# An attention and two-mixer kernel: finishing additions spread over the second mixer, angle products between its halves, the first result ahead of the token sums, two half blocks, and a later hold on GpSimd

## What is computed

```python
attn_out = local_and_global_attention(q, k, v)        # 8 heads of 64, window 96, 8 global keys
x = attn_out.transpose(0, 2, 1, 3).reshape(B, S, 512)
# first mixer
h  = np.maximum(x.transpose(0, 2, 1) @ w_tok1, 0.0) @ w_tok2     # 768 -> 256 -> 768
u  = x + h.transpose(0, 2, 1)
x2 = u + np.maximum(u @ w_ch1, 0.0) @ w_ch2                      # 512 -> 1536 -> 512
# second mixer
theta = x2 @ w_theta
y   = einsum('ts,bsd->btd', w_tok_r, x2 * cos(theta)) + einsum('ts,bsd->btd', w_tok_i, x2 * sin(theta))
u2  = x2 + y
out = u2 + np.maximum(u2 @ w_ch, 0.0)
```

## Time and profile before

| | us |
|---|---|
| median of 3 runs (lowest, highest) | 514.46 (514.01, 514.79) |
| profiled execution, its own time | 514.55 |
| span of the profiled execution, first to last instruction | 512.8 |
| PE busy in it | 491.1 (96%) |
| DVE busy | 326.4 (64%) |
| POOL busy | 265.7 (52%) |
| ACT busy | 192.9 (38%) |
| mean granted PE clock | 0.993 of 2.4 GHz |

### The profile page before, as it was taken

How to read it: one execution, slowest core, us unless ns; L and a number is a source line. 1 busy time by engine, 2 the same in 40 slices (tenths; PEclk the granted TensorE clock), 3 DMA queues, 4 the chain that set the end, 5 groups by cost and what they waited for, 6 DMA issues and landing times.

```text
span 512.8 us, 8394 instructions
## 1 busy us (share of the span) xinstructions
PE 491.1 (96%) x2917; PEld 445.3 (87%) x2917; DVE 326.4 (64%) x797; ACT 192.9 (38%) x413; POOL 265.7 (52%) x315
## 2 busy tenths in 40 slices
PE   7999999999999999998899999994999999999997
PEld 5999999898999999797799989883778899888897
DVE  6998998577434353587423346898587684664452
ACT  6999899454111131154111114342232140321130
POOL 3575566599589884069998882473450130000040
PEclk9999999999999999999999999997999999999999
DMA  6897775422222331103143241223001221000002
GB/s 231 316 310 239 230 221 132 133 82 84 65 83 81 98 115 54 42 0 122 43 111 118 78 128 61 93 93 102 23 21 36 69 82 63 0 1 0 2 31 93
DMA packets 27083, 49.81 MB, mean 97 GB/s; under 512 B 3360, under 2 KB 17696, under 8 KB 27040
## 3 DMA queue, kind: packets, MB, share of 16 engines
q1 hardware_dynamic: 27040, 49.26, 30.6%
HBM read 39.81 MB, written 3.15 MB: 84 GB/s over the span
## 4 chain that ended last, share of the span: by engine, by line
PE 84%; POOL 5%; DVE 5%; issue 3%; DMA 1%; ACT 1%; POOLq 0%; DVEq 0%
PE bank L323 61%; PE bank L1758 7%; PE bank L1486 5%; PE bank L1516 4%; PE bank L1519 3%; POOL wsplit L710 3%; PE bank L1500 2%; PE bank L1498 2%; POOL wsplit L704 1%; DMA wraw<-weights 1%; DVE split L1279 1%; DMA counts<-both_counts 1%; DVE bank L1308 1%; PE bank L1526 0%; DVE act_raw L1209 0%
## 5 line engine op out<-in xcount | busy, mean ns | idle before, releaser
L323 PE MATMUL bank<-wsplit 128*128 128x512 f32 (+2 forms) x816 | 149.0, 338 | 1.7 <-DVE bank L1297 1.7
L323 PEld LDWEIGHTS bank<-wsplit 128*128 128x128 f32 x816 | 134.4, 188 | 15.7 <-POOL wsplit L710 1.1
L710 POOL TENSOR_TENSOR wsplit<-wraw,wsplit 128x512 fp32r<-128x512 f32 (+1 forms) x77 | 100.4, 1305 | 39.4 <-ACT wsplit L883 33.8
L323 PE MATMUL bank<-wsplit,zs 128*128 128x512 f32 (+1 forms) x576 | 103.2, 338 | 0.0
L323 PEld LDWEIGHTS bank<-wsplit,zs 128*128 128x128 f32 x576 | 89.6, 188 | 14.1 <-issue 0.2
L778 POOL TENSOR_TENSOR split<-act_raw,split 128x384 fp32r<-128x384 f32 x12 | 12.5, 1075 | 106.4 <-ACT split L995 106.4
L323 PE MATMUL bank<-split,wsplit 128*128 128x384 f32 x276 | 55.1, 342 | 3.3 <-POOL wsplit L710 1.6
L652 POOL TENSOR_TENSOR wsplit<-qk_raw,wsplit 64x256 fp32r<-64x256 f32 x46 | 38.0, 827 | 33.9 <-DVE wsplit L1038 33.5
L323 PEld LDWEIGHTS bank<-split,wsplit 128*128 128x128 f32 x276 | 46.8, 188 | 5.9 <-issue 2.5
L704 POOL CAST wsplit<-wraw 128x512 fp32r<-128x512 f32 (+1 forms) x59 | 36.1, 613 | 28.6 <-PE bank L323 19.2
L323 PE MATMUL bank<-wsplit,tile 128*128 128x512 f32 x144 | 37.6, 412 | 9.6 <-issue 9.3
(11 more groups left out here) (126 smaller groups left out, 749.3 us busy)
## 6 DMA issues: line engine op xcount, KB each, us to landing
wraw<-weights SPq DMA_DIRECT2D x28, 512.0 KB, 3.4
qk_raw<-qk SPq DMA_DIRECT2D x23, 528.0 KB, 4.5
wraw<-weights SPq DMA_DIRECT2D x8, 768.0 KB, 4.0
vt<-v SPq DMA_DIRECT2D x10, 520.0 KB, 4.7
xT<-turned SPq DMA_DIRECT2D x64, 48.0 KB, 2.0
out<-act_raw SPq DMA_DIRECT2D x16, 192.0 KB, 1.9
xT<-turned_early SPq DMA_DIRECT2D x16, 96.0 KB, 2.5
xT<-wraw SPq DMA_DIRECT2D x32, 48.0 KB, 2.0
```

The lines of the kernel that those rows point to most:

```text
L323: mm = pe.matmul(dst, lhs(a), rhs(c), start=first and i == 0, stop=last and i == 2, skip_group_check=True)
L710: ins = pool.tensor_tensor(dst[:, cols], src[:, cols], hi[:, cols].bitcast(F32), ALU.subtract)
```

## The change

Five edits of order. The number and sizes of the instructions stay the same, on every engine; nothing is computed otherwise.

1. *Finishing additions.* Of batch 1's eight, three stay where they were; the other five go behind the low part of the first half of tile 2 (`z_to_lo(2, 0)`).
2. *Angle products.* In batch 0, `angles(g+2)` goes from ahead of `mix(g)` to between its halves.
3. *First result.* On DVE, `result_to_lo(0)` goes ahead of the first token sums, and the next result follows two sums later; on ACT, result i+1 is rounded ahead of sums 2i and 2i+1. Result 3 goes behind the last two `find_sum`.
4. *Two half blocks.* Sum t = 4 goes to banks 0 and 1. Of pair 0's blocks, d = 2 and 3 come first, and of each only the part of 512 columns (banks 2 and 3, which then wait for no sum) stands behind product 0 of pair 1; their parts of 256 columns stand behind product 1.
5. *GpSimd's hold.* POOL's wait for `x2_done` goes from ahead of chunk 16 to behind its combinations and roundings, ahead of its subtractions.

```diff
-            return bank[{1: 4, 3: 0, 2: 4, 4: 2}[t] + kk][:, 0:SC]
+            return bank[{1: 4, 3: 0, 2: 4, 4: 0}[t] + kk][:, 0:SC]
...
                 round_in_pieces(mixes(n, 0, 3, MIXES), sums)
+                if n == PAIR_F + 1:
+                    pool.wait_ge(x2_done, NC * KD)
                 link(rest_in_pieces(mixes(n, 1, 0, 3), raw[:, 0:3 * 2 * P], mixes(n, 0, 0, 3)))
...
-                        if n == PAIR_F + 1:
-                            pool.wait_ge(x2_done, NC * KD)
                         split_first(n, raw).then_inc(w_ready, 1)
...
-                for i, (f, c) in enumerate(REGULAR):
+                def result_to_hi(i):
+                    f, c = REGULAR[i]
                     act.wait_ge(r1_ready, b * PRODUCTS + i + 1)
                     act.activation(r1_at(b * PAIR_F, f, 0, c * SC, SC), bank[6 + i % 2][:, 0:SC],
                                    ACT.Relu).then_inc(r1_hi, 1)
+
+                result_to_hi(0)
+                for i in range(len(REGULAR)):
+                    if i + 1 < len(REGULAR):
+                        result_to_hi(i + 1)
                     sum_to_hi(2 * i)
                     sum_to_hi(2 * i + 1)
...
                         dve.wait_ge(t_hi, b * SUMS + 5 + kk)
+                        dve.wait_ge(t_lo, b * SUMS + 3 + kk)
+                        dve.wait_ge(t_raw, b * SUMS + 5 + kk)
                         src, raw_u, op = t_psum(2, kk), u_raw[:, 2 + kk], ALU.subtract
...
+                result_to_lo(0)
+                for i in range(len(REGULAR)):
+                    find_sum(2 * i)
+                    find_sum(2 * i + 1)
                     if i < 2:
-                        sum_to_lo(2 * i)
-                        sum_to_lo(2 * i + 1)
-                    elif i == 2:
-                        sum_to_lo(4)
-                    else:
-                        sum_to_lo(5)
-                        find_sum(6)
-                        find_sum(7)
-                        sum_to_lo(6)
-                        sum_to_lo(7)
+                        result_to_lo(i + 1)
+                    elif i == 3:
+                        result_to_lo(3)
+                    sum_to_lo(2 * i)
+                    sum_to_lo(2 * i + 1)
...
             z_to_lo(1, 0)
             tile_to_lo(B * T + 3)
-            for i in range(2 * KD):
+            for i in range(3):
                 finish_x2(B - 1, i)
...
                     if g >= 2 and not (b and s == 0):
                         z_to_lo(g, 0)
+                    if g == 2:
+                        for i in range(3, 2 * KD):
+                            finish_x2(B - 1, i)
...
-                def block(i, f, d):
+                def first_block(i, f, d, at):
                     n = b * PAIR_F + i
                     first, last = i == 0 and f == 0, i == PAIR_F - 1 and f == 0
-                    if d == 0:
+                    if d == at:
                         wait_weight(pair_in_order(b, i, 1))
                         pe.wait_ge(r1_lo, b * PARTS + 2 * NC * i + (3 + f if i == 0 else 4 - f))
-                    if first:
-                        pe.wait_ge(t_lo, b * SUMS + 5 + d)
-                        pe.wait_ge(t_raw, b * SUMS + 7 + d // 2)
-                    three(pe, bank[d][:, :], lambda a: second_at(n, a, f * DM + d * P, P),
-                          lambda a: r1_at(n, f, a, 0, 512), first, last)
+                    if first and d < 2:
+                        pe.wait_ge(t_lo, b * SUMS + 7 + d)
+                    return three(pe, bank[d][:, :], lambda a: second_at(n, a, f * DM + d * P, P),
+                                 lambda a: r1_at(n, f, a, 0, 512), first, last)
+
+                def rest_of_block(i, f, d):
+                    n = b * PAIR_F + i
+                    first, last = i == 0 and f == 0, i == PAIR_F - 1 and f == 0
+                    if first and d == 2:
+                        pe.wait_ge(t_lo, b * SUMS + 6)
+                        pe.wait_ge(t_raw, b * SUMS + 8)
                     mm = three(pe, bank[4 + d // 2][:, d % 2 * 256:(d % 2 + 1) * 256],
...
+                    if i == 1:
+                        blocks = blocks[2:4] + blocks[0:2] + blocks[4:]
...
-                block(i - 1, *blocks[2 if ahead else 0])
+                    if i == 1:
+                        first_block(0, *blocks[0], 2)
+                        first_block(0, *blocks[1], 2)
+                    else:
+                        block(i - 1, *blocks[2 if ahead else 0])
                     pe.wait_ge(p1_copied, m + 1)
                     product(i, 1, 6, quarter(2, 0), True)
-                    block(i - 1, *blocks[3 if ahead else 1])
+                    if i == 1:
+                        rest_of_block(0, *blocks[0])
+                        rest_of_block(0, *blocks[1])
+                    else:
+                        block(i - 1, *blocks[3 if ahead else 1])
...
                     mm.then_inc(z_used, 1)
+                    if b == 0 and i == 0 and s + 2 < T:
+                        angles(g + 2)
...
                     g = b * T + s
-                    if b == 0 and s + 2 < T:
-                        angles(g + 2)
```

9 lines of the change are left out of this document (5 added, 4 removed).

## The result

The kernel after took 503.19 us (median of 4 executions, 501.59 to 503.63) against 514.62 us for the kernel before, measured on the same chip: a ratio of 0.9771, with a 95% interval of 0.9746 to 0.9797. That is 11.4 us less; forecast were 9.2 us and 505.3 us.

The account below looks back on a forecast made before the run. The prediction took PE to bound the kernel, busy 491.1 of 512.8 us. Gains of 6.4 + 1.2 + 1.6 = 9.2 us took the profiled 514.55 to 505.35, 505.3 against the median; range 502.8 to 508.5.

Parts of the forecast that it names:

- What bounds the kernel: Whole span: PE busy 491.1 of 512.8 us, so only its gaps and slow stretches can give time.
- Edits 1 and 2, the work: Second mixer's start on PE: 12 halves and four angle products take 62.1 us, against 71.0 before.
- Edits 1 and 2, the waits: Second mixer, PE waiting for DVE at tiles 3 and 4: 2.1 to 4.4 us, taken as 2.5.
- two before POOL comes back, 0.9 us, three beside it, 1.75 + 2 x 1.44, to 361.4: DVE's five moved additions, from 355.8: two at full pace, three slowed by POOL, ending at 361.4.
- rival A: Second mixer: DVE keeps up, fewer instructions meeting POOL, waits near nothing; 502.8, up to 504 us; chance 0.15.
- Rival C: Clock falls in or after the new 2.7 us wait ahead of mix(0), costing 1.8 us: 507.1; chance 0.07.
- Edits 3 and 4: First mixer, first result and half blocks: 0.7 us gained in batch 1 and 0.5 in batch 0, 1.2 together.
- Edit 5: First mixer, batch 1: chunk 20 ready earlier, PE's whole wait of 1.61 us goes; gain 1.6 us.
- Rival D: At chunk 20 another wait (a load) replaces the hold and PE still stands: 506.9 us; chance 0.04.
- Rival E: Slower or level: clock falls ahead of mix(0) and stays low through short waits; 515.5 us; chance 0.05.

Follow-up runs that it names:

- both mixer edits: Kernel before with only five finishing additions moved back and angle products placed between the halves of the mixes; 506.83 us, ratio 0.9828.
- the hold alone: Kernel before with only POOL's wait for x2_done moved behind chunk 16's combinations and roundings; 512.51 us, ratio 0.9953.
- the first-mixer edits: Kernel before with only the first result ahead of the sums and two half blocks ahead of the copy; 513.92 us, ratio 0.9976.
- the last kernel: Kernel after with ACT's copy earlier, tile 2's angle product first, tile 5's behind tile 3's product, additions behind tile 3's low halves; 498.54 us, ratio 0.9675.

## Why the prediction was right, and where it was not

The time fell inside the range and 2.1 us under the forecast. By its steps:

- **What bounds the kernel** held: all but 0.8 us of the span's 13.0 came out of PE's gaps and slow matmuls in the four places named.
- **Edits 1 and 2, the work** held to 0.1 us: 62.1 forecast, 62.2 measured, 2.56 us of new wait ahead of it against 2.7. DVE was laid out almost to the row: the moved additions were put at 355.8 and POOL's return at 356.7, and with both edits alone they came at 355.85 and 356.94.
- **Edits 1 and 2, the waits** is the term that was mis-sized, 2.5 us for none. The step that failed is "two before POOL comes back, 0.9 us, three beside it, 1.75 + 2 x 1.44, to 361.4". All five took 2.29 and ended at 358.1. That 5.6 us were forecast and the run that puts all five behind POOL's start took 5.71 is chance: the forecast had two of the five clear of POOL, and by its prices, 1.75 and 1.44, five beside POOL would take 7.8. Its price held for the two beside subtractions (1.78 and 1.77), while beside casts the three took 0.8 each. And the price depends on who was there first: the prediction took POOL's arrival as the moment from which DVE pays, and it was POOL that paid. So rival A came about in the profiled execution, by another way than it named: not fewer meetings, but meetings that DVE won; the sign named for A, additions of under 1 us beside a working POOL, is in the trace (0.46). With the additions behind POOL's start, the executions at full clock were 2.1 to 2.2 us longer, near the 2.5 forecast: this supports that the waits would have come, had POOL been first.
- **The clock** was the other error, of the opposite sign. Rival C, at 0.07, happened, by the mean clocks, in three of four executions of after and in three of five with both mixer edits; of the six traces with a wait of 2.56 to 2.60 ahead of `mix(0)`, five show the fall. Its price was about right: 1.8 forecast, 503.2 - 501.6 = 1.6 and 506.9 - 505.0 = 1.9 measured between executions, 1.3 to 1.5 on the traces. The argument against it (the clock had held for 5.0 us of idling before) drew a rule from one execution: in the same gap of 7.8 us it fell 2.3 us after PE had stopped in the trace of the hold alone, and 2.4 us after in that of the first-mixer edits. The two errors leave 8.9 - 1.6 = 7.3 us in the median against 6.4 forecast; that they nearly cancel is luck.
- **Edits 3 and 4**: 1.55 us measured in the profiles, 1.2 forecast. The wait for result 0 (0.37, forecast 0.3) and the work ahead of the copy held. With edits 3 and 4 alone PE resumed product 1 at 239.08 against 240.48, 1.4 us earlier, of which 0.2 was there before any edit, 0.65 stems from batch 0 and 0.54 from batch 1; forecast were 0.5 and 0.4. Alone, the gain was nearly lost to the clock, a way in which neither forecast nor rivals had it.
- **Edit 5**: 1.6 forecast, 1.8 on both traces, 2.3 by the time of the edit alone (interval 1.7 to 3.2). POOL's wait, 11.02 us, is what it was to be (near 11). The wait row of 1.61 counts only the idle matmul engine; from row to row the place cost 3.87 us before and 2.10 without the wait, 1.77. Rival D didn't come about.
- **The edits together**: the three groups alone gave 2.3 + 7.9 + 0.9 = 11.1 us, together 11.4. Within the intervals the groups add up, though edit 5 also protects what edits 3 and 4 gain. Within the mixer group they overlap nearly whole, which the prediction, having priced both edits as one, didn't say.
- Rival E found no support: in every trace the clock was full again within 5 us of PE's going back to work.
- **What no term covers**: 0.6 of the 13.0 us of span lie at the start and the end, outside all edits, so that much of the 2.1 us below the forecast is put down to the executions and not to the change.

What stays open: what decides, from one execution to the next, whether the clock falls in a wait of 2 to 3 us. The runs show only where it did.

## What to carry to other kernels

Lay out by hand both the engine that waits and the one that releases, and ask of every wait that you cover how much slack the next release has: here covering 2.56 us of wait gained next to nothing (0.4 us by the medians, inside the noise), since the releasing engine had 0.9 us left. Two edits that lengthen the same distance are worth one of them; time the pair with one taken back before keeping both. And when a copy stands in a queue behind work that waits for another engine, as ACT's did behind the last sums, moving it ahead is a few lines and was worth 3.7 us here, more than edits 3, 4 and 5 by their own runs (0.9 and 2.3).

## What the runs showed of the hardware that was not expected

**The shared port goes by who holds it.** Three additions that met a working POOL took 4.92 us in the kernel after too (from 335.82), whereas the five back to back took 2.30 with POOL's piece starting among them. They were followed without a break by a low half:

```profile
354.05 0.68 DVE L1249 TENSOR_TENSOR zs<-zb,zs 128x512 fp32r<-128x512 f32 x1
```

POOL's piece, 352.89 to 355.88, would have needed 1.35 us, so it began in fact at about 354.5 (worked out, not seen), as this low half was ending. The Trainium skill ("SBUF — State Buffer", section "SBUF: two separate sides") says that of two such instructions whichever starts first holds the port pair that DVE and GpSimd share, for its whole length, and the other blocks. The rows agree on the blocking and show more than one instruction: DVE kept the pair over a run of them, for some 1.6 us. Where POOL had started first, neither side kept it: DVE's five took 5.71 us, and POOL's two subtractions 3.03 instead of 2.66. In both runs the five are the same instructions, two of 512 columns and three of 256, so width doesn't separate them.

**The clock fell in or behind waits of 1.87 to 3.3 us in most traces, and held for about 5 us of idling in another.** In the profiled runs it fell at waits of 3.26, 2.56 to 2.60 (five times), 2.28, 2.15 and 1.87 us, between 0.6 us before PE resumed and 1.5 us after. At the kernel after's own wait of 2.56 it held. In the gap of 7.8 us it fell 4.8 us after PE's last matmul had ended in the kernel before, and 2.3 and 2.4 us after in two others. A spell cost 1.3 to 1.6 us at the shorter waits and 1.8 to 2.2 us behind the gap of 7.8, from start to start on the traces. In the last kernel, whose longest wait in the second mixer is 1.18 us, the mean clock was 1.00 in all five executions.
